# Loads and stores at the three seams of a convolution-and-MLP kernel: positions first, weights loaded and split in the middle stage, smaller first and last transfers

## What is computed

```python
h_filt = (np.maximum(pos_emb @ w1, 0.0) @ w2) * np.exp(-0.01 * pos)[:, None]
u = x * v
L = 2 * S
y = irfft(rfft(u, n=L, axis=1) * rfft(h_filt, n=L, axis=0)[None], n=L, axis=1)[:, :S, :]
t = (x * y).reshape(B * S, D)
h = t @ w_in
P = a[0] + a[1] * h + a[2] * h**2 + a[3] * h**3
Q = 1.0 + abs(b[0]) * abs(h) + abs(b[1]) * h**2
out = (P / (Q + 1e-06)) @ w_out
```

## Time and profile before

| what | value |
|---|---|
| median of 3 runs | 2112.35 us (2111.99 to 2113.26) |
| the profiled execution | 2115.88 us, its span 2114.1 us |
| stage 1, PE's first to last matmul | 11.4 to 234.3 us |
| PE idle between stage 1 and stage 2 | 26.85 us |
| stage 2, PE's first to last matmul | 261.1 to about 602.8 us |
| PE idle between stage 2 and stage 3 | 14.26 us |
| stage 3 | 617.0 us to the end |
| busy share of the span | PE 94%, POOL 89%, DVE 86%, ACT 86% |

### The profile page before, as it was taken

How to read it: one execution, slowest core, us unless ns; L and a number is a source line. 1 busy time by engine, 2 the same in 40 slices (tenths; PEclk the granted TensorE clock), 3 DMA queues, 4 the chain that set the end, 5 groups by cost and what they waited for, 6 DMA issues and landing times. The chain is left out here.

```text
span 2114.1 us, 33039 instructions
## 1 busy us (share of the span) xinstructions
PE 1985.2 (94%) x8964; PEld 1467.0 (69%) x8964; DVE 1827.0 (86%) x2511; ACT 1826.1 (86%) x2671; POOL 1872.4 (89%) x1218
## 2 busy tenths in 40 slices
PE   6999499999969999999999999999999999999998
PEld 4767399999956666666666666666666666666664
DVE  4888488888848999999999989999899999999997
ACT  4888466666638999999999999999999999999998
POOL 3777388888829999999999989999999999999997
PEclk9999799999979999999999999999999999999999
DMA  6999856776650111111111111111111111111100
GB/s 172 299 303 313 229 141 171 182 176 171 165 124 2 36 32 32 41 48 34 32 32 32 32 33 32 32 36 32 33 32 47 44 32 32 32 32 32 32 13 13
DMA packets 65843, 176.34 MB, mean 83 GB/s; under 512 B 5046, under 2 KB 8414, under 8 KB 62686
## 3 DMA queue, kind: packets, MB, share of 16 engines
q1 hardware_dynamic: 65694, 174.67, 30.6%
HBM read 102.89 MB, written 71.76 MB: 83 GB/s over the span
## 5 line engine op out<-in xcount | busy, mean ns | idle before, releaser
L636 POOL TENSOR_TENSOR den<-slope,mag 128x832 f32<-128x832 f32 x480 | 947.9, 1975 | 0.0
L885 PE MATMUL acc_p<-g_s,w_out_k 128*128 128x416 f32 x1920 | 769.5, 523 | 49.6 <-DVE oT L807 24.5
L766 DVE SCALAR_TENSOR_TENSOR num<-square,level,h_p 128x832 f32<-128x832 f32 x480 | 518.1, 1079 | 83.0 <-ACT square L674 43.6
L628 POOL TENSOR_SCALAR slope<-mag,den_c 128x832 f32<-128x832 f32 x480 | 499.8, 1041 | 80.6 <-DVE mag L761 51.1
L885 PEld LDWEIGHTS acc_p<-g_s,w_out_k 128*128 128x128 f32 x1920 | 341.5, 189 | 296.2 <-issue 183.5
L799 DVE SCALAR_TENSOR_TENSOR g_s<-num,ratio,r_p 128x832 f32<-128x832 f32 x480 | 518.1, 1079 | 20.3 <-ACT r_p L690 5.8
L674 ACT ACTIVATE square<-h_p,centre 128x832 f32<-128x832 f32 x480 | 470.5, 980 | 41.8 <-issue 21.0
L874 PE MATMUL h_p<-xy_hi,w_lo 128*128 128x416 f32 x960 | 460.8, 480 | 7.1 <-DVE num L766 4.5
L683 ACT ACTIVATE den<-den 128x832 f32<-128x832 f32 x480 | 442.9, 923 | 6.9 <-POOL den L636 6.8
L690 ACT ACTIVATE r_p<-den 128x832 f32<-128x832 f32 x480 | 428.6, 893 | 0.9 <-DVE g_s L799 0.7
L874 PE MATMUL h_p<-xy_lo,w_hi 128*128 128x416 f32 x960 | 338.6, 353 | 0.0
(11 more groups left out here) (79 smaller groups left out, 2806.3 us busy)
## 6 DMA issues: line engine op xcount, KB each, us to landing
bent<-bent_s SPq DMA_DIRECT2D x60, 576.0 KB, 6.9
bin_s<-bent SPq DMA_DIRECT2D x24, 1440.0 KB, 9.8
x_s<-in_x SPq DMA_DIRECT2D x60, 416.0 KB
back<-back_s SPq DMA_DIRECT2D x24, 960.0 KB, 7.8
vin_s<-back SPq DMA_DIRECT2D x30, 768.0 KB, 6.2
v_s<-in_v SPq DMA_DIRECT2D x30, 416.0 KB
out<-o_s SPq DMA_DIRECT2D x60, 208.0 KB
pos_s<-in_pos_emb SPq DMA_DIRECT2D x30, 88.0 KB
```

The lines of the kernel that those rows point to most:

```text
L628: nc.gpsimd.tensor_scalar(slope[:, q % DEEP], mag[:, q % DEEP], den_c[:, 1:2], den_c[:, 0:1], ALU.mult, ALU.add).then_inc(slope_done, 1)
L636: nc.gpsimd.tensor_tensor(den[:, q % DEEP], slope[:, q % DEEP], mag[:, q % DEEP], ALU.mult).then_inc(den_done, 1)
L766: nc.vector.scalar_tensor_tensor(out=num[:, q % NUMS], in0=square[:, q % SQUARES], scalar=level[:], in1=h_p[:, q % 2, :, 0:TOK], op0=ALU.a ...
L885: mm = nc.tensor.matmul(acc_p[:, 0:TOK], w_out_k[:, ft], g_s[:, q % DEEP, t], start=(ft == 0), stop=(ft == FT - 1))
```

## The change

Four edits, all in where and when data is loaded, stored or split; no arithmetic on the data differs.

1. Stage 1: in `load` the positions are issued ahead of x and v, after the wait for the transposes alone; x and v keep their wait for the product.
2. `unfold`, `w_in`, `w_out`, `coef` and `den_raw` move from SP's list at the end of stage 1 into stage 2, behind the loads of its first two blocks and ahead of the third. `w_hi` and `w_lo` move from the start of stage 2 to behind its last bin on ACT and on DVE.
3. Stage 2: the first block of bins is loaded in four transfers of one k, each with a semaphore of its own (`first_in`), and the last block is stored in four transfers of one k (`last_out`).
4. Stage 3: the first block of `back` and x is loaded in two halves (`first_vin`, `first_x`).

```diff
                 def load(i, q):
                     blk, s = i * PER + q, q % SLOTS
                     if positive(blk - 1):
+                        sp.wait_ge(posT_ps, blk - 1)
+                    sp.dma_start(pos_s[:, s], pos_r[:, bass.ds(blk * JB, JB), :]).then_inc(pos_in[s], 16)
+                    if positive(blk - 1):
                         sp.wait_ge(prod_done, blk - 1)
-                        sp.wait_ge(posT_ps, blk - 1)
                     sp.dma_start(x_s[:, s], x_r[:, :, bass.ds(blk * JB, JB), :]).then_inc(xv_in[s], 16)
                     sp.dma_start(v_s[:, s], v_r[:, :, bass.ds(blk * JB, JB), :]).then_inc(xv_in[s], 16)
-                    sp.dma_start(pos_s[:, s], pos_r[:, bass.ds(blk * JB, JB), :]).then_inc(pos_in[s], 16)
...
+                for k in range(JB):
+                    sp.dma_start(bin_s[:, 0, k].rearrange("p c f -> p (c f)"), bent[k]).then_inc(first_in[k], 16)
+                load(1, 1)
+                for dst, src in ((coef, a.rearrange("(o n) -> o n", o=1).to_broadcast([128, 4])),
+                                 (den_raw, b.rearrange("(o n) -> o n", o=1).to_broadcast([128, 2])),
+                                 (unfold_s, tab["unfold"]), (w_in_s, w_in),
+                                 (w_out_s, w_out.rearrange("(t p) d -> p t d", p=128))):
+                    sp.dma_start(dst[:], src).then_inc(later_in, 16)
                 AHEAD = SLOTS + 1
-                for blk in range(AHEAD):
-                    load(blk, blk % SLOTS)
+                load(2, 0)
...
+                for m in range(JB):
+                    k = (K_BLOCKS - 1) * JB + m
+                    sp.wait_ge(vturned[k % 2], k // 2 + 1)
+                    sp.dma_start(back[:, k], back_s[:, (K_BLOCKS - 1) % SLOTS, m].rearrange("p c f -> p (c f)")
+                                 ).then_inc(last_out, 16)
...
+                act.wait_ge(spread_in, SPREAD)
+                nc.scalar.activation(spread_hi[:], spread_s[:], ACT.Copy).then_inc(split_done, 1)
+                pipelined(act, ITERS, PER, [(LEAD_MULT, filter_copy), (LEAD_SPLIT, split_bin), (LEAD_Y, split_y), (0, cos_part)])
                 act.wait_ge(later_in, LATER)
-                nc.scalar.activation(spread_hi[:], spread_s[:], ACT.Copy).then_inc(split_done, 1)
                 nc.scalar.activation(w_hi[:], w_in_s[:], ACT.Copy).then_inc(split_done, 1)
-                pipelined(act, ITERS, PER, [(LEAD_MULT, filter_copy), (LEAD_SPLIT, split_bin), (LEAD_Y, split_y), (0, cos_part)])
...
-                load(0, 0)
+                for half in range(2):
+                    j = slice(half * HALF, (half + 1) * HALF)
+                    sp.dma_start(vin_s[:, 0, j].rearrange("p j c f -> p j (c f)"),
+                                 back[j].rearrange("j k f -> k j f")).then_inc(first_vin[half], 16)
+                    for b_ in range(BATCH):
+                        sp.dma_start(x_s[:, 0, b_, j], x_r[:, b_, j]).then_inc(first_x[half], 16)
                 load(1, 1)
```

More of the change, by code:

```diff
@@ L123, in hyena_mlp @@
         den_raw = kept("den_raw", [128, 2])
-        later_in, split_done = sem("later_in"), sem("split_done")
-        LATER = 16 * 7
+        spread_in, later_in, split_done = sem("spread_in"), sem("later_in"), sem("split_done")
+        SPREAD, LATER = 16 * 2, 16 * 5
         with ExitStack() as ctx:
@@ L192, in _ @@
                 pipelined(sp, ITERS, PER, [(0, store), (LEAD_LOAD, load)])
[L193 to L197, removed]
+                for dst, src in ((spread_s, tab["spread"]), (turn_j, tab["turn_j"])):
+                    sp.dma_start(dst[:], src).then_inc(spread_in, 16)
                 for out_sem in bent_out:
@@ L407, in _ @@
                         store(i * SLOTS + s, s)
-                for blk in range((ITERS - SLOTS) * SLOTS, K_BLOCKS):
+                for blk in range((ITERS - SLOTS) * SLOTS, K_BLOCKS - 1):
                     if blk + AHEAD < K_BLOCKS:
@@ L411, in _ @@
                     store(blk, blk % SLOTS)
+                for m in range(JB):
[3 more added lines that the diff above has]
+                                 ).then_inc(last_out, 16)
                 for s in range(SLOTS):
-                    sp.wait_ge(back_out[s], 16 * ITERS)
+                    sp.wait_ge(back_out[s], 16 * (ITERS - s))
+                sp.wait_ge(last_out, 16 * JB)
             @block.gpsimd
@@ L435, in split_bin @@
                     s, m = q // JB, q % JB
-                    if m == 0:
-                        act.wait_ge(bin_in[s], 16 * (i + 1))
+                    if isinstance(k, int) and k < JB:
+                        act.wait_ge(first_in[k], 16)
+                    elif m == 0:
+                        act.wait_ge(bin_in[s], 16 * (i + s))
                     if positive(k - BINS + 1):
@@ L494, in turn @@
                                                    ).then_inc(vturned[q % 2], 1)
-                dve.wait_ge(split_done, 4)
+                dve.wait_ge(split_done, 3)
                 nc.vector.tensor_tensor(spread_lo[:], spread_s[:], spread_hi[:].bitcast(F32), ALU.subtract).then_inc(split_done, 1)
+                pipelined(dve, ITERS, PER, [(LEAD_MULT, multiply), (0, turn)])
+                dve.wait_ge(split_done, 5)
                 nc.vector.tensor_tensor(w_lo[:], w_in_s[:], w_hi[:].bitcast(F32), ALU.subtract).then_inc(split_done, 1)
-                pipelined(dve, ITERS, PER, [(LEAD_MULT, multiply), (0, turn)])
             @block.tensor
@@ L578, in hyena_mlp @@
             vin_in, x_in = sems("vin_in"), sems("x_in")
+            first_vin, first_x = sems("first_vin"), sems("first_x")
             rows_done, xy_done, xyT_done = sem("rows_done"), sem("xy_done"), sem("xyT_done")
@@ L740, in times_x @@
                     dve.wait_ge(rows_done, n + 1)
-                    if half == 0:
-                        dve.wait_ge(x_in[s], 16 * (i + 1))
+                    if isinstance(n, int) and n < 2:
+                        dve.wait_ge(first_x[half], 16 * BATCH)
+                    elif half == 0:
+                        dve.wait_ge(x_in[s], 16 * (i + s))
                     if positive(n):
@@ L846, in rows @@
                 def rows(n, i, s, half, freed):
-                    if half == 0:
-                        pe.wait_ge(vin_in[s], 16 * (i + 1))
+                    if isinstance(n, int) and n < 2:
+                        pe.wait_ge(first_vin[half], 16)
+                    elif half == 0:
+                        pe.wait_ge(vin_in[s], 16 * (i + s))
                     freed()
```

4 lines of the change are left out of this document (2 added, 2 removed).

## The result

| | kernel before | kernel after |
|---|---|---|
| median of the timed runs beside each other | 2112.81 us (2111.99 to 2114.63, 4 runs) | 2089.46 us (2086.96 to 2089.76, 4 runs) |
| ratio | | 0.9888, 95% interval [0.9874, 0.9903] |
| the profiled execution, its span | 2115.88 us, 2114.1 us | 2086.96 us, 2084.5 us |

The change takes 23.35 us off the median; 2091 us was forecast.

What follows compares the result with a forecast made beforehand. PE bounds stage 2 and POOL stage 3, leaving PE's waits at the start, both seams and stage 1's loop. Terms -4.0 - 2.9 - 12.5 + 2.2 - 4.2 = -21.4 us gave 2091 us from the median, range 2086 to 2098.

Steps and rivals of the forecast that it cites:

- Start: Start of stage 1: positions first lets the first transposes start near 6.7 and `filt` run at 12.4; -4.0 us.
- the worse bound of -2.2: Start of stage 1: the gain if PE's clock rise does not move with the work, so more runs at half rate.
- Loop of stage 1: Stage 1's later blocks: transposes stop waiting for positions, which are issued about 3 us earlier; -2.9 us, bounds -2.9 and 0.
- First seam: Between stages 1 and 2: bins issued at 241.4, ACT starts k 0 at 245.75 instead of 258.25; -12.5 us.
- a single k 1.85 + 2.4: First seam: one k of bins takes 1.85 us of transfer plus 2.4 of fixed latency, 4.25 in all.
- Rival (b): First bins: the four k transfers each pay 2.4 us latency, k 4 stalls PE by 7; 2098 us, chance 0.05.
- Third block of bins: Early stage 2: this block, queued behind the weights, lands 3.9 us late for ACT; +2.2 us reaches PE, bounds 0 to +6.
- I take 9.0 between: Early stage 2: five weight transfers take 9.0 us, between 8.3 by bytes and 9.4 for seven; bounds 6.8 and 12.8.
- Rival (a): Early stage 2: weights hide, block 2 not late through PE's slack and faster weights; -23.6 us, 2089, chance 0.13.
- Second seam: Between stages 2 and 3: store by k -2.4 us, half of `vin_s` -1.8; PE starts stage 3 4.2 us earlier.
- Stage 3: Last stage: the change touches none of its instructions but the first load; 0 us forecast.
- Rival (c): Loop of stage 1: positions first does nothing, the wait moves to x and v; -18.5 us, 2094, chance 0.10.

Runs made afterwards that it cites:

- pos_only: Kernel before with only the positions loaded ahead of x and v in stage 1; 2108.08 us, ratio 0.9975.
- undo_pos: Changed kernel with x and v loaded ahead of the positions again; 2094.34 us, ratio 0.9916 of the kernel before.
- whole_first: Changed kernel with the first block of bins in one transfer again; 2097.09 us, ratio 0.9927 of the kernel before.
- weights_before_block1: Changed kernel with the five weight transfers ahead of the second block of bins, still behind k 0 to 3; 2099.15 us, ratio 0.9940 of the kernel before.
- whole_vin: Changed kernel with the first load of stage 3 whole again; 2090.56 us, ratio 0.9902 of the kernel before.
- The three parts alone: Kernel before with edit 1 alone, edit 2 alone, or edits 3 and 4 alone; ratios 0.9975, 0.9971 and 0.9949.

## Why the prediction was right

The time, the sign and the order of the terms held: the first seam is more than half of the gain. That the total came within 1.5 us of the measured time is in part luck: one term gave 2.1 us less than forecast, the others together 5.3 more. Term by term:

- **Start, -4.0 forecast, -4.7 in the profile pair.** The fourth transposes move by 4.8 in pos_only and 4.3 in undo_pos. First transposes at 6.67 (6.7 forecast) and `filt` at 12.08 (12.4). The clock's rise moved with the work (the first fold matmul of 0.34 us starts at 32.0 in place of 36.5), so the worse bound of -2.2 was not met; PE's first transposes now wait for the table `fold_lo` on DVE, not for a load.
- **Loop of stage 1, -2.9 forecast, about -0.8.** This term was mis-sized. Its working took the one profile of before as what the kernel always does. Six profiles in the old order give 178.92, 179.31, 179.47, 179.68, 180.18 and 181.74 us, mean 179.9; eight in the new one 178.8 to 179.5, mean 179.1. The forecast's profile was the worst of the six. The wait for positions does go away, as it said; mostly it was hardly there. Even in the forecast's profile PE's four waits for positions add up to 1.2 us only, not to the 2.9 that the step put down to them; what else lengthened that one execution is open.
- **First seam, -12.5 forecast, -13.7.** The bins are issued 6.8 us after PE's last fold matmul (7.1 forecast). The prediction speaks of five more transfers to issue and did not see that one of them, `coef`, took 5.36 us of SP. The first k lands 3.4 us after issue, not 4.25: "a single k 1.85 + 2.4" was too dear. Rival (b), latencies that add up, would put block 1 another 7.2 us back; it lands 14.0 us after its issue, with four transfers of one k ahead of it. Of the two prices that the prediction set side by side for k 0, measured against the same issue, 4.25 from the rows and 2.8 by the Trainium skill, DMA: Bandwidth & Descriptors, section "Anatomy of one DMA", the 3.4 lies in the middle. The Trainium skill gives that formula for transfers issued by GpSimd; SP issues these. The rule to coalesce of the Trainium skill, DMA: Bandwidth & Descriptors, section "Rules for kernel authors", is one for bandwidth. It does not serve the first transfer of a stage here: whole_first, which follows it, costs 8.2 us.
- **Third block of bins, +2.2 forecast, 0.** The step "I take 9.0 between" failed: the five weight transfers take 6.7 us here, just under the lower bound of 6.8 (behind the single k, in weights_before_block1, they take 9.7). With block 1 also earlier, block 2 comes 1.14 us late for ACT, and PE's slack covers that. Rival (a), the weights hide, was right on this term. weights_before_block1 shows that they are hidden by their place only.
- **Second seam, -4.2 forecast, -5.4.** Store and split: -2.8 against -2.4, with the last rotation's 3.51 us to the first load, of which 0.6 is the split. The half of `vin_s`: -2.7 in the profile pair and -2.1 by whole_vin, against -1.8: the byte rate of the earlier trace rows, 216 GB/s, was too fast for it. The half lands 3.5 us after issue and the whole 5.7 (whole_vin) to 6.2 us (the kernel before), so 0.39 MB took 2.2 to 2.7 us, an estimate of 145 to 180 GB/s.
- **Stage 3, 0 forecast.** -3.1 in the profile pair, and not shown to be the change's by any timed run.

So the loop gave 2.1 us less than forecast, and the start 0.7, the third block 2.2 and the two seams 2.4 us more: 3.2 in all, which makes -24.6 of the forecast's -21.4. The medians say -23.35 and the ratio -23.7, between -20.5 and -26.6; the forecast time of 2091 us is 1.5 us above the median. Rival (c), 2094 us, was nearer in the size of the loop's term, but not for its reason: the wait did not move to x and v, it was seldom there.

The three parts alone give -5.3, -6.1 and -10.8, together -22.2 us, against -23.7 by the ratio of the whole; the intervals are wider than the difference, but the first seam's gap, read in the traces, does show 2.7 us that only both edits together bring.

What stays open: why the engines stand 1.5 us at a turn of stage 3's loop in one profile and 2.6 in another. I did not try a stage 3 without a loop. The Trainium skill, Runtime: NRT & Kernel Launch, section "Instruction fetch mechanics", says that a branch taken to a target outside what has been fetched stalls the engine. A stand of all engines at a loop's turn, put down to "issue" in ACT's row of the kernel after (in the kernel before, to POOL's `den`), would fit that; no run here shows that it is the cause.

## What to carry to other kernels

At a seam where all engines meet, ask what the first compute instruction needs, make that the first and smallest transfer, and put what a later stage needs only behind as many of the next stage's loads as PE would otherwise wait for; then test the place, since one block further forward cost 11 us here. Work taken from a seam's start to its end is not free: check what becomes the last thing (here the weight split, 0.6 us), and whether it runs beside a GpSimd operation. Behind a transfer of many small rows look at how long the next issue takes: here it held SP, and with it the end of the stage, for 5.4 us. A wait of a few us that comes from one profile is a sample: look at a second execution before it goes into a sum.

## What I had not expected of the hardware

- DVE and GpSimd hold each other up: `bin_lo` 3.5 us in place of 1.86 beside `w_lo`, and a quarter of `w_lo` 1.60 in place of 0.67 beside `y_lo`.
- The issue behind the 2048 rows of `w_out` holds SP: 5.36 us before, 8.10 in weights_before_block1, against 0.3 to 0.5 for most.
- Four transfers of 360 KB in a row cost no added latency that shows: the first lands 3.4 us after issue, and the block behind them is there 15.7 us after the first issue (233.84 to 249.6). In whole_first, at the same place, the second of two whole blocks takes 17.7 (issued 234.17, 0.4 us behind the first, 17.3 us to landing).
- PE's wait of 7.4 us in weights_before_block1 came with a stage 2 that is 11.0 longer, as PE came out of it at half clock.
- Two profiles of one and the same kernel differ by 2.8 us in the loop of stage 1 (181.74 and 178.92).
